# Four later rounds of a token routing: the threshold by sorting instead of by counting search, and a smaller first piece for the first expert

## The chip, the cores and the metric

The kernel runs on one core of one Trainium2 chip. The metric is the device time of the whole kernel in microseconds, as the median of several executions. A profile is one execution of its own; its times are counted from the first instruction (the span's start). The core has a matrix engine (TensorE, "PE" in the rows, with its weight loads as "PEld"), a vector engine (VectorE, "DVE"), a scalar engine (ScalarE, "ACT"), a general engine (GpSimd, "POOL") and an engine that here only issues transfers (SyncE, "SP"). Each runs its own list of instructions in order, and they meet at semaphores.

## The reference

```python
x = attention(q, k, v, f_logit)            # gated linear recurrence, then (3072 tokens, 384)
# routing and first network
cap = N // E                               # 3072 // 8 = 384
logits = x @ w_gate                        # (3072, 8)
for idx in np.argsort(-logits.flatten()):  # greedy, best logit first
    tok, e = idx // E, idx % E
    if assigned[tok] >= 0 or counts[e] >= cap: continue
    assigned[tok] = e; counts[e] += 1
for e in range(E):
    out[assigned == e] = np.maximum(x[assigned == e] @ w1[e], 0.0) @ w2[e]
# second network on every token: h = x @ w_in; g = h * clip(h + 3, 0, 6) / 6; y = g @ w_out
```

With 384 places in each of 8 experts and 3072 tokens, the greedy loop ends with every expert exactly full. The kernel computes the same assignment in rounds: every token picks the best expert that is left to it, every expert finds the logit of its 384th best token (its threshold), the tokens below it lose that expert and pick again. When no expert is over 384, the choice is the reference's.

## The kernel before

**Stages.** First the attention, in 24 units of 128 tokens, on all engines, with the weights of the second network split into a high and a low part beside it (chunks of 512 columns, loaded by SP, rounded by ScalarE, the rest subtracted by GpSimd). It leaves the 24 x 8 logits of each of the 128 lanes in `logit` (128 x 192). Then the routing. Then 8 experts one after the other, each with 384 gathered tokens: transpose, first network, second network, scatter of the result. Every product there is three matmuls (high x high, high x low, low x high; lines 1580 to 1582).

**A routing round** (`for r in range(COARSE)`, line 1238, four rounds with `DIGITS = (3, 3, 4, 4)`). `make_values` (L1099) writes to `vm` the logit of each token's choice and about -1e38 elsewhere. VectorE (L1104, tiles 0 to 8) and ScalarE (L811, tiles 9 to 23) copy `vm` to `vsel`, each value 16 times; TensorE turns the 24 tiles (`turn_values`, L1506), so that PSUM lane 16 e + j holds all 3072 values of expert e, for 16 trial keys j. Then comes the search, 3 or 4 digits of base 16 long. For each digit VectorE counts the values at or above the lane's key in the first 1408 columns (L1179), ScalarE in the other 1664 (L814), L1187 compares the sum with 384, a matmul (L1535) adds up the lanes' verdicts, and L1205 makes the next key. The last key is the threshold (`base`); `threshold` (L1521) brings it to all lanes. `limit_choice` (L1077, L1080) drops the logits under it, `choose` (L1086, L1089) finds each token's new best expert. From the second round on a search starts at the key found in the round before it, with a window of a 16th of the scale (`set_window`, L1129 to L1136).

TensorE also runs matmuls whose results nobody reads: `warm` (L1494, 128 columns each) and 16 others of 128 columns ahead of a round's last digit (L1533).

**After the rounds** `count_choice` (L1514, L1516) and `judge` (L1147 to L1174) count each expert's tokens and work out where each token stands in its expert's list. If an expert is still over 384, `exact_rounds` runs further rounds, with eight digits each, behind a flag that all engines read (`load_flag`). 24 matmuls (L1573) sum the row numbers, L1297 writes `ids`, and GpSimd gathers the rows of expert 0 in three indirect transfers of 128 rows (L682).

**Expert 0's start.** TensorE turns tile 0 as it lands (`first_turn`, L1597), ScalarE and VectorE split it in high and low (L864, L1306), then `first_hidden(0)` multiplies it with the first two 128-column blocks of w1 (18 matmuls of 128 columns). Only then are tiles 1 and 2 turned and split, and `first_hidden(1)` and `first_hidden(2)` follow, with 18 matmuls of 128 columns each. Afterwards `expert` goes on with `hidden(2)`, which waits for the first block's low part (`hl`, L1312, behind `hh`, L872).

**Weights of expert 0.** SP loads w1[0] (L544) when the attention's stores have landed and w2[0] (L547) when w1[0] has been split, both through one buffer `raw`. GpSimd splits both in six pieces of 512 columns (L671 and L673), with waits on `v_turned` that hold pieces back to the second and third round. `expert_split` must be through before `first_hidden`. The end of the kernel is GpSimd's wait for all 24 scatters (L721).

Of the kernel before, what the change touches and what calls it, by code (L numbers as in the profile page):

```python
# [4 lines left out]
F32 = mybir.dt.float32  # L5
# [3 lines left out]
I32 = mybir.dt.int32  # L9
U32 = mybir.dt.uint32  # L10
ALU = mybir.AluOpType
# [33 lines left out]
DIGITS = (3, 3, 4, 4)  # L45
WINDOW = 1.0 / 16.0
COARSE = len(DIGITS)
BEFORE = tuple(sum(DIGITS[:r]) for r in range(COARSE + 1))
COARSE_STEPS = BEFORE[COARSE]
# [4 lines left out]
def build(nc, q, k, v, f, wg, w1, w2, wi, wo, out):  # L54
    ctx = ExitStack()
    with ctx:
# [61 lines left out]
        bottom = place("acts", "bottom", [P, 1])  # L118
        wide_lane = place("acts", "wide_lane", [P, 1])
        window = place("acts", "window", [P, 1])  # L120
# [20 lines left out]
        count_from = place("acts", "count_from", [P, 1])  # L141
        count_a = place("acts", "count_a", [P, 1])
# [51 lines left out]
        vm = place("routing", "vm", [P, NT, NE])  # L194
# [43 lines left out]
        w2h = place("expert", "w2h", [P, F1 // P, DM], F32R)  # L238
        w2l = place("expert", "w2l", [P, F1 // P, DM], F32R)
# [11 lines left out]
        count_d, unread = psum[:, ND + 16:ND + 17], p7[:, 0:P]  # L251
# [4 lines left out]
        id_ps = p5[:, 0:NT]  # L256
        fT_ps, kT_ps, qT_ps = p0, p1, p2
# [75 lines left out]
        order_counted = sem("order_counted")  # L333
        placing = sem("placing")
# [7 lines left out]
        window_set = sem("window_set")  # L342
        moves_set = sem("moves_set")
# [4 lines left out]
        raw_loaded = sem("raw_loaded")  # L348
        high_done = sem("high_done")
# [130 lines left out]
        def exact_key(r):  # L480
            return (STEPS - 1) * (r - COARSE) + COARSE_STEPS - COARSE

# [3 lines left out]
        def _(sp):  # L486
# [52 lines left out]
            def weights(e):  # L539
                if first(e):  # L540
                    sp.wait_ge(chunk_split, NT)
                else:
                    sp.wait_ge(split_done, 2 * e)
# [6 lines left out]
            def exact():  # L550
# [13 lines left out]
                sp.wait_ge(scan_stored, 1 + 16 * NT)  # L564
            for i in range(B):
                sp.wait_ge(x_stored[i], 16 * TT)
# [3 lines left out]
            weights(0)  # L570
# [4 lines left out]
            experts(sp, expert)  # L575

        @block.gpsimd
        def _(pool):
# [11 lines left out]
            for i in range(MOST):  # L590
# [6 lines left out]
                               pattern=[[16, NE], [0, 16]], channel_multiplier=-1).then_inc(rc, 1)  # L597
            pool.memset(head[:, :], 0.0).then_inc(rc, 1)
# [57 lines left out]
            def split(q, high, low):  # L656

                pool.wait_ge(raw_loaded, 16 * q + 16)
                high = high.rearrange("p c n -> p (c n)")
                low = low.rearrange("p c n -> p (c n)")  # L660
                pieces = PIECES if q < 2 else 1
                size = 3072 // pieces
                for i in range(pieces):
# [3 lines left out]
                    if q == 0 and i == 4:  # L667
                        pool.wait_ge(v_turned, 2)
# [1049 lines left out]
```

## Time and profile before

| | |
|---|---|
| median of 3 runs | 885.61 us (885.39 to 890.78) |
| the profiled execution | 886.32 us |
| its span, first to last instruction | 883.8 us |
| TensorE busy | 825.5 us (93% of the span) |
| VectorE, ScalarE, GpSimd busy | 384.3, 346.7, 324.8 us |
| chain that ended last, by engine | PE 89%, DVE 6%, issue 2%, the rest 3% |

A row of the chain gives start, length and what ran (`x2` means two instructions merged). A row of a timeline gives start, busy time, engine, line, operation, output and inputs with their shapes, and in brackets how long the engine had been idle and what ended that. A fp32 matmul appears as two. "PEclk" is the clock that TensorE was granted, 1.00 being its upper level (2.4 GHz) and 0.50 its lower one (1.2 GHz); a number between them is a mean over both.

### The profile page before, as it was taken

What the parts mean: (1) busy time and instruction counts of PE and PEld (TensorE: products, weight loads), DVE (VectorE), ACT (ScalarE), POOL (GpSimd) and SP (SyncE); (2) the same over time, 40 slices, a digit from 0 to 9 for tenths busy, and PEclk for the clock granted to TensorE, in tenths of its full rate; (3) what the DMA queues carried; (4) which work ended last, traced back from release to release, by engine and by line L of the source; (5) the groups of instructions that cost most, each with busy time, mean ns of one, the idle gap of its engine ahead of it and who ended that gap; (6) DMA issues with size and microseconds to landing.
All of it is one profiled execution on the core that took longest, in us unless ns stands there. A gap on an engine that the chain in (4) does not pass through costs nothing.

```text
span 883.8 us, 15679 instructions
## 1 busy us (share of the span) xinstructions
PE 825.5 (93%) x6030; PEld 795.6 (90%) x6030; DVE 384.3 (43%) x717; ACT 346.7 (39%) x631; POOL 324.8 (37%) x249
## 2 busy tenths in 40 slices
PE   5999999965569999999999999999999999999995
PEld 4899989854459999999999999999999999999995
DVE  6778776556741442343143234324313322431331
ACT  4766766444521432333143233314323332432332
POOL 4676767634220522440161244116024422601001
PEclk8999999977679999999999999999999999999998
DMA  9999999322210221040121103012211200200000
GB/s 164 200 175 186 184 193 173 79 83 71 72 36 20 72 72 54 1 143 10 45 71 71 53 6 136 19 34 71 71 53 36 106 30 23 71 0 27 1 1 27
DMA packets 126806, 65.03 MB, mean 74 GB/s; under 512 B 102448, under 2 KB 119856, under 8 KB 126768
## 3 DMA queue, kind: packets, MB, share of 16 engines
q1 hardware_dynamic: 123696, 55.09, 28.8%
q0 software_dynamic: 3072, 9.44, 3.3%
q8 instruction: 24, 0.39, 0.2%
q14 instruction: 14, 0.11, 0.0%
HBM read 55.07 MB, written 9.44 MB: 73 GB/s over the span
## 4 chain that ended last, share of the span: by engine, by line
PE 89%; DVE 6%; issue 2%; SPq 1%; ACT 1%; DMA 1%; POOL 0%; DVEq 0%; POOLq 0%
PE psum L1580 23%; PE psum L1582 22%; PE psum L1581 22%; PE psum L1340 4%; PE psum L1392 3%; DVE junk L1179 3%; PE psum L1427 3%; PE psum L1442 2%; PE psum L1377 2%; PE psum L1506 2%; PE psum L1405 1%; PE psum L1435 1%; PE psum L1369 1%; SPq L499 1%; PE psum L1591 1%
## 5 line engine op out<-in xcount | busy, mean ns | idle before, releaser
L1322 DVE SCALAR_TENSOR_TENSOR psum<-rg,psum 128x384 f32<-128x384 f32 x128 | 72.0, 563 | 155.3 <-ACT rg L882 155.3
L882 ACT ACTIVATE rg<-psum,three 128x384 f32<-128x384 f32 x128 | 74.5, 582 | 153.1 <-PE psum L1582 153.1
L1580 PE MATMUL psum<-yh,w_high 128*128 128x384 f32 x384 | 130.7, 340 | 0.9
L1580 PE MATMUL psum<-w_high,gh 128*128 128x384 f32 x384 | 128.4, 334 | 0.3 <-DVE gl L1325 0.3
L1582 PE MATMUL psum<-yh,w_low 128*128 128x384 f32 x384 | 128.6, 335 | 0.0
L1581 PE MATMUL psum<-yl,w_high 128*128 128x384 f32 x384 | 128.5, 335 | 0.0
L1582 PE MATMUL psum<-w_high,gl 128*128 128x384 f32 x384 | 128.3, 334 | 0.0
L1581 PE MATMUL psum<-w_low,gh 128*128 128x384 f32 x384 | 128.3, 334 | 0.0
L716 POOL DMA_INDIRECT out_dram<-ys,ids x24 | 24.1, 1002 | 255.2 <-ACT ys L897 250.6
L1312 DVE SCALAR_TENSOR_TENSOR hl<-psum,hh 128x384 fp32r<-128x384 f32 x64 | 35.7, 558 | 166.2 <-ACT hh L872 166.2
L1325 DVE SCALAR_TENSOR_TENSOR gl<-psum,gh 128x384 fp32r<-128x384 f32 x128 | 71.4, 558 | 72.4 <-ACT gh L886 72.4
L886 ACT ACTIVATE gh<-psum 128x384 fp32r<-128x384 f32 x128 | 63.0, 493 | 81.5 <-DVE psum L1322 81.5
L872 ACT ACTIVATE hh<-psum 128x384 fp32r<-128x384 f32 x64 | 31.5, 492 | 146.3 <-PE psum L1582 142.8
L671 POOL CAST w1h<-raw 128x3072 fp32r<-128x3072 f32 (+1 forms) x13 | 22.9, 1764 | 145.0 <-PE psum L1582 125.8
L1580 PEld LDWEIGHTS psum<-yh,w_high 128*128 128x128 f32 x384 | 72.1, 188 | 4.3 <-DVE yl L1316 3.5
L1580 PEld LDWEIGHTS psum<-w_high,gh 128*128 128x128 f32 x384 | 72.1, 188 | 0.6 <-DVE gl L1325 0.6
L1581 PEld LDWEIGHTS psum<-yl,w_high 128*128 128x128 f32 x384 | 72.2, 188 | 0.0
L1582 PEld LDWEIGHTS psum<-w_high,gl 128*128 128x128 f32 x384 | 72.1, 188 | 0.0
L1581 PEld LDWEIGHTS psum<-w_low,gh 128*128 128x128 f32 x384 | 72.1, 188 | 0.0
L1582 PEld LDWEIGHTS psum<-yh,w_low 128*128 128x128 f32 x384 | 72.1, 188 | 0.0
L1580 PE MATMUL psum<-xh,w1h 128*128 128x384 f32 (+1 forms) x204 | 67.3, 330 | 1.8 <-DVE xl L1306 1.6
L1582 PE MATMUL psum<-xh,w1l 128*128 128x384 f32 (+1 forms) x204 | 67.2, 329 | 0.0
(191 smaller groups left out, 1616.1 us busy)
## 6 DMA issues: line engine op xcount, KB each, us to landing
raw<-in_moe_w_dram SPq DMA_DIRECT2D x16, 1536.0 KB, 6.5
f_in<-in_f_logit_dram SPq DMA_DIRECT2D x24, 192.0 KB, 4.6
k_in<-in_k_dram SPq DMA_DIRECT2D x24, 192.0 KB, 5.2
q_in<-in_q_dram SPq DMA_DIRECT2D x24, 192.0 KB, 5.5
v_in<-in_v_dram SPq DMA_DIRECT2D x24, 192.0 KB, 4.6
x_rows<-x_nat SPq DMA_DIRECT2D x24, 192.0 KB, 4.1
raw<-in_moe_w_in_dram SPq DMA_DIRECT2D x12, 256.0 KB, 4.3
raw<-in_moe_w_out_dram SPq DMA_DIRECT2D x12, 256.0 KB, 3.4
```

The costliest lines, as they stand in the source:

```text
L872: act.activation(hh[:, j % 2, :], banks[j % 2][:, 0:CAP], ACT.Relu).then_inc(hh_done, 1)
L882: act.activation(rg[:, j % 2, :], banks[j % 3][:, 0:CAP], ACT.Relu, bias=three[:, 0:1]).then_inc(r_done, 1)
L886: act.mul(gh[:, j % 3, :], banks[j % 3][:, 0:CAP], 1.0 / 6.0).then_inc(gh_done, 1)
L1179: dve.tensor_scalar(junk[:, :], v_dve, key, count_from[:, 0:1], ALU.is_ge, ALU.add, accum_out=count_d).then_inc(count_done, 1)
L1312: dve.scalar_tensor_tensor(out=hl[:, j % 2, :], in0=banks[j % 2][:, 0:CAP], scalar=0.0, in1=hh[:, j % 2, :].bitcast(F32), op0=ALU.max, op1 ...
L1322: dve.scalar_tensor_tensor(out=bank, in0=rg[:, j % 2, :], scalar=6.0, in1=bank, op0=ALU.min, op1=ALU.mult).then_inc(gg_done, 1)
L1325: dve.scalar_tensor_tensor(out=gl[:, j % 3, :], in0=bank, scalar=1.0 / 6.0, in1=gh[:, j % 3, :].bitcast(F32), op0=ALU.mult, op1=ALU.subtra ...
L1340: last = pe.transpose(dst[:, P * g:P * g + P], src[:, b, 2 * g:2 * g + 2, :].rearrange("p a b -> p (a b)"), ident[:, :])
L1392: last = pe.matmul(a_ps[j][:, P * g:P * g + P], k_sc[r, i, P * g:P * g + P], q_sc[r, i, P * g:P * g + P], start=True, stop=True)
L1580: pe.matmul(bank, high, rhs_high, start=start, stop=False)
L1581: pe.matmul(bank, high, rhs_low, start=False, stop=False)
L1582: return pe.matmul(bank, low, rhs_high, start=False, stop=stop)
```

## The change

Round 1 stays a search, with two digits instead of three. It is followed by four rounds of another kind (`RANKED = 4`; five rounds in all). In such a round `vm` holds the negated logit of the choice, and about -1e38 elsewhere, in 32 tiles (24 and 8 that are always empty). Four transposes without any widening turn it, two to bank 0 and two to bank 1 (`ranked_ps`, `ranked_too`), so that a lane holds 256 values of one expert. VectorE takes the eight largest of each lane (`dve.max`; the negated values make them the eight smallest logits), copies them to a 16 x 8 grid in which only the lane's own tile is not zero (`spread`), and a matmul with `lane_expert` collects the 128 candidates of each expert in one lane (`merged_ps`). A second `dve.max` sorts out the eight smallest of the expert. ScalarE counts each lane's chosen tokens with one pass over `ranked_too` (as printed), a matmul sums the lanes of an expert, and VectorE picks from the eight the entry that belongs to the number of tokens over 384. A round can so drop at most seven tokens of an expert. TensorE runs 9 matmuls of 512 columns per such round whose results nobody reads (`fill`).

Further parts: w1[0] is loaded as soon as the attention's chunks are split; w2[0] goes to a place of its own (`w2_raw`, over `w2l`) once round 1 has turned its values; its high part is made by ScalarE in the ranked rounds, two pieces in each of the first three, its low part by GpSimd. GpSimd reads the gathers' bound from a register that is set once. `first_hidden` multiplies tile 0 alone with block 0, then with block 1, then tiles 1 and 2 together. The wait for the last scatters goes from GpSimd to SP. Small tables are made at the kernel's start, and one of VectorE's table steps waits for them.

```diff
-DIGITS = (3, 3, 4, 4)
+DIGITS = (2,)
+SEARCHED = len(DIGITS)
+RANKED = 4
+W2_ROUND = ((0, 2), (2, 4), (4, 6), (6, 6))
...
 sp
-                if first(e):
-                    sp.wait_ge(chunk_split, NT)
...
+            sp.wait_ge(chunk_split, NT)
+            sp.dma_start(raw[:, :]..., w1[0:1, :, :]...).then_inc(raw_loaded, 16)
             for i in range(B):
                 sp.wait_ge(x_stored[i], 16 * TT)
...
-            weights(0)
+            sp.wait_ge(v_turned, 1)
+            sp.dma_start(w2_raw[:, :]..., w2[0:1, :, :]...).then_inc(w2_loaded, 16)
...
+            sp.wait_ge(stored, 48 * NE)
 pool
-                    if q == 0 and i == 4:
-                        pool.wait_ge(v_turned, 2)
-                    if q == 1 and i == 0:
-                        pool.wait_ge(v_turned, 3)
...
+            pool.reg_mov(last_row, NTOK - 1)
...
-                                            bounds_check=NTOK - 1, oob_is_err=False).then_inc(xs_loaded[t], 16)
+                                            bounds_check=last_row, oob_is_err=False).then_inc(xs_loaded[t], 16)
...
-            expert_split(0)
+            split(0, w1h[:, :, :], w1l[:, :, :])
+            for i in range(PIECES):
+                finish_w2(i)          # waits for w2_high, subtracts
+            pool.wait_ge(w2_low, PIECES)
+            pool.sem_inc(split_done, 1)
...
-            pool.wait_ge(stored, 48 * NE)
 act
+            act.wait_ge(rank_tables, 3)
+            for r in range(1, RANKED + 1):
+                act.wait_ge(ranked_turned_too, r)
+                act.activation(junk_a[:, 0:2 * P], ranked_too, ACT.Sign, scale=1.0, bias=half_big[:, 0:1],
+                               accum_out=lane_count[:, :]).then_inc(lane_counted, 1)
+                for i in range(*W2_ROUND[r - 1]):
+                    if i == 0:
+                        act.wait_ge(w2_loaded, 16)
+                    act.copy(w2h[...][:, at], w2_raw[:, at]).then_inc(w2_high, 1)
 dve
+            def make_ranked(r):
+                dve.scalar_tensor_tensor(out=flat(vm[:, :, :]), in0=low_ps, scalar=-BIG, in1=flat(logit[:, :, :]),
+                                         op0=ALU.mult, op1=ALU.subtract).then_inc(ranked_made, 1)
+            def rank(r):
+                dve.wait_ge(ranked_turned, r)
+                dve.max(out=top_ps, in_=ranked_ps).then_inc(top_done, 1)
+                dve.wait_ge(top_done, r)
+                dve.tensor_tensor(spread[...], top_ps..., lane_tile..., ALU.mult).then_inc(spread_done, 1)
+                dve.wait_ge(merged, r)
+                dve.max(out=least_ps[:, 1:RANKS + 1], in_=merged_ps).then_inc(sorted_done, 1)
+                dve.wait_ge(lanes_summed, r)
+                dve.tensor_scalar(code_ps, lane_sum_ps, rank_code_at(RANKS - 1), rank_code_at(-1), ALU.min, ALU.max).then_inc(code_done, 1)
+                dve.wait_ge(code_done, r)
+                dve.wait_ge(sorted_done, r)
+                dve.scalar_tensor_tensor(out=picked[:, :], in0=rank_code[0:NE, :], scalar=code_ps, in1=least_ps, op0=ALU.is_equal,
+                                         op1=ALU.mult, accum_out=least[:, :]).then_inc(least_done, 1)
...
-            for r in range(COARSE):
+            for r in range(SEARCHED):
                 make_values(r)
-                if r == 0:
-                    set_scale()
-                else:
-                    set_window(r)
+                set_scale()
+                ranked_constants()    # minus (8 x 8), and a memset of vm's empty tiles
                 coarse(r)
+                limit_choice(r)
+                choose(r + 1)
+            dve.memset(least_ps[:, 0:1], BIG)
+            for r in range(1, RANKED + 1):
+                make_ranked(r)
+                rank(r)
                 limit_choice(r)
                 choose(r + 1)
 pe
+            def rank(r):
+                fill(p4, 4 * P, 5)
+                pe.wait_ge(ranked_made, r)
+                ...
+                for dst_ps, done in ((ranked_ps, ranked_turned), (ranked_too, ranked_turned_too)):
+                    for i in range(2):
+                        last = pe.transpose(...)
+                    last.then_inc(done, 1)
+                fill(p4, 4 * P, 2)
+                pe.wait_ge(spread_done, r)
+                pe.matmul(merged_ps, lane_expert[:, :], spread[:, :], start=True, stop=True).then_inc(merged, 1)
+                pe.wait_ge(lane_counted, r)
+                pe.matmul(lane_sum_ps, lane_expert[:, :], lane_count[:, :], start=True, stop=True).then_inc(lanes_summed, 1)
+                fill(p4, 4 * P, 2)
+                pe.wait_ge(least_done, r)
+                pe.matmul(thr_ps, least[:, 0:1].broadcast_to([NE, P]), minus[:, :], start=True, stop=True).then_inc(t_ready, 1)
...
-            warm(16)
             pe.wait_ge(x_copied, NT)
+            fill(p0, 4 * P, 2)
             pe.wait_ge(measured, 2)
             pe.matmul(peak_ps, peak[:, 0:1], ident[:, :], start=True, stop=True).then_inc(peak_turned, 1)
+            fill(p0, 4 * P, 4)
...
-                    if i and i == DIGITS[r] - 1:
+                    if i:
                         pe.wait_ge(bits_ready, BEFORE[r] - r + i)
-                        for _ in range(16):
-                            pe.matmul(unread, ones_b[:, :], ones_b[:, :], start=True, stop=True)
+                    else:
+                        pe.wait_ge(scaled, 1)
+                    fill(p7, 3 * P, 8)
...
             first_turn(0)
-            warm_late(2)
-            pe.wait_ge(ids_known, 1)
-            pe.wait_ge(split_done, 2)
-            first_hidden(0)
             first_turn(1)
+            pe.wait_ge(split_done, 1)
+            first_hidden(0, 1, 0)
             first_turn(2)
-            first_hidden(1)
-            first_hidden(2)
+            first_hidden(0, 1, 1)
+            first_hidden(1, 3, 0)
+            first_hidden(1, 3, 1)
```

## Rows read from the trace of the kernel before

**Rows 1.** Windows: stretch, length, busy us (count) by engine, PEclk, DMA share, GB/s.
```profile
253.80:267.10 13.30, 10.02 (x83) 9.28 (x81) 2.14 (x4) 1.94 (x5) 6.25 (x6) 0.99 0.26 77
267.10:875.50 608.40, 606.64 (x3501) 602.11 (x3501) 201.15 (x364) 199.15 (x388) 174.66 (x68) 1.00 0.14 47
```

**Rows 2.** Chain that ended last, round 1, the start of round 2, and round 4's end.
```profile
187.96 1.82 DVE junk L1179 x2
...
190.57 1.82 DVE junk L1179 x2
...
193.20 0.61 PE psum L1521 x2
193.84 0.38 DVE psum L1077
...
196.23 4.44 PE psum L1506 x24
...
243.74 0.38 DVE psum L1077
```

**Rows 3.** Groups of VectorE in the routing, 178 to 253 us: busy, mean ns.
```profile
L1179 DVE TENSOR_SCALAR_CACHE_REDUCE junk<-psum,coarse_key,count_from 128x1408 bf16<-128x1408 f32 x10 | 17.4, 1744 | 0.4
...
L1077 DVE TENSOR_TENSOR psum<-logit_peak,psum 128x192 f32<-128x192 f32 x4 | 1.5, 364 | 2.8 <-PE psum L1521 2.8
...
L1086 DVE TENSOR_REDUCE psum<-logit_peak 128x24 f32<-128x192 f32 x4 | 1.4, 361 | 0.1
...
L1153 DVE TENSOR_REDUCE slotf<-incl 128x24 f32<-128x192 f32 x1 | 0.6, 615 | 0.0
```

**Rows 4.** Chain: four transposes, and the matmul that turns the peak.
```profile
174.97 0.66 PE psum L1369 x4
...
180.06 0.51 PE psum L1526 x2
```

**Rows 5.** Timeline of TensorE, the unread matmuls ahead of a last digit.
```profile
190.59 1.89 PE L1533 MATMUL psum<-ones_b 128*128 128x128 bf16 x16 [0.39 <-DVE coarse_key L1205]
```

**Rows 6.** Windows, columns as in rows 1: end of round 1, round 2's transposes, its first count.
```profile
189.70:196.20 6.50, 5.39 (x42) 4.28 (x42) 4.94 (x16) 2.13 (x3) 3.95 (x5) 0.50 0.00 0
196.20:199.80 3.60, 3.57 (x18) 3.57 (x19) 1.15 (x6) 1.59 (x3) 0.00 (x0) 0.54 0.02 5
200.00:203.20 3.20, 0.84 (x8) 0.53 (x5) 2.11 (x5) 1.74 (x2) 2.40 (x3) 0.96 0.00 0
```

**Rows 7.** Groups of ScalarE in 180 to 330 us: busy, mean ns.
```profile
L811 ACT COPY vsel<-vm 128x640 f32<-128x640 f32 x10 | 6.7, 722 | 10.5 <-DVE vm L1099 10.5
...
L886 ACT ACTIVATE gh<-psum 128x384 fp32r<-128x384 f32 x13 | 6.4, 493 | 8.2 <-DVE psum L1322 8.2
...
L814 ACT ACTIVATION_READ_ACCUMULATOR junk_a<-psum,coarse_key 128x1 f32 x10 | 1.9, 193 | 0.0
```

**Rows 8.** Timeline of GpSimd: first piece of w1[0], last piece of w2[0].
```profile
186.16 0.61 POOL L671 CAST w1h<-raw 128x512 fp32r<-128x512 f32 x1 [12.32 <-DMA raw<-in_moe_w_dram]
...
225.59 1.27 POOL L673 TENSOR_TENSOR w2l<-raw,w2h 128x512 fp32r<-128x512 f32 x1
```

**Rows 9.** Chain from the token lists to the first expert's steady work.
```profile
252.61 0.19 DVE ids L1297
...
253.77 3.40 DMA xs<-x_rows,ids
257.21 0.56 PE psum L1597 x3
...
259.01 0.30 PE psum L1580
...
265.98 0.50 ACT hh L872
...
267.12 0.44 PE psum L1580
267.56 0.17 PE psum L1581
```

More of the change, by code:

```diff
@@ L44 @@
 UNCHOSEN = 4096.0
-DIGITS = (3, 3, 4, 4)
[L46 to L49, printed above, removed]
+DIGITS = (2,)
+SEARCHED = len(DIGITS)
+RANKED = 4
+COARSE = SEARCHED + RANKED
+BEFORE = tuple(sum(DIGITS[:r]) for r in range(SEARCHED + 1))
+COARSE_STEPS = BEFORE[SEARCHED]
+LANE_TILES = 16
+RANKS = 8
+W2_ROUND = ((0, 2), (2, 4), (4, 6), (6, 6))
 MOST = max(DIGITS)
@@ L193, in build @@
         junk_a = place("routing", "junk_a", [P, NTOK - ND], BF16)
-        vm = place("routing", "vm", [P, NT, NE])
+        vm_all = place("routing", "vm_all", [P, 2 * LANE_TILES, NE])
+        vm = vm_all[:, 0:NT, :]
         vsel = place("routing", "vsel", [P, NT, NE, 16])
@@ L238, in build @@
         w2h = place("expert", "w2h", [P, F1 // P, DM], F32R)
+        top["w2 raw"], limit["w2 raw"] = top["expert"], limit["expert"]
+        w2_raw = place("w2 raw", "w2_raw", [P, F1 // P * DM])
         w2l = place("expert", "w2l", [P, F1 // P, DM], F32R)
@@ L250, in build @@
         digit_ps, thr_ps = p7[:, 384:385], p7[:, 392:392 + NE]
[L251 removed]
+        count_d = psum[:, ND + 16:ND + 17]
         def value_at(n):
@@ L842, in search @@
                 widen_rest(r)
-                act.wait_ge(v_turned, r + 1)
+                act.wait_ge(v_turned, turning(r) + 1)
                 for i in range(STEPS):
@@ L1176, in judge, with test @@
                                       ALU.is_equal).then_inc(columns_done, 1)
-            def test(key, m, starts=None):
+            def test(key, m):
                 dve.tensor_scalar(junk[:, :], v_dve, key, count_from[:, 0:1], ALU.is_ge, ALU.add,
                                   accum_out=count_d).then_inc(count_done, 1)
-                if starts is not None:
-                    size = scale if starts == 0 else window
-                    dve.tensor_scalar(move_ps, unit_move[:, :], size[:, 0:1], None, ALU.mult).then_inc(moves_set, 1)
-                    dve.wait_ge(moves_set, starts + 1)
+                if isinstance(m, int) and m == 0:
+                    dve.tensor_scalar(move_ps, unit_move[:, :], scale[:, 0:1], None, ALU.mult).then_inc(scaled, 1)
+                    dve.wait_ge(scaled, 4)
                 dve.wait_ge(count_done, m + 1)
@@ L1190, in coarse @@
             def coarse(r):
-                dve.wait_ge(v_turned, r + 1)
+                dve.wait_ge(v_turned, turning(r) + 1)
                 for i in range(DIGITS[r]):
@@ L1208, in search @@
             def search(r):
-                dve.wait_ge(v_turned, r + 1)
+                dve.wait_ge(v_turned, turning(r) + 1)
                 for i in range(STEPS):
@@ L1519, in threshold, with fill @@
             def threshold(r):
-                pe.wait_ge(base_done, r + 1)
+                pe.wait_ge(base_done, turning(r) + 1)
                 pe.matmul(thr_ps, base[:, 0:1].bitcast(F32).broadcast_to([P, P]), head[:, :], start=True, stop=True).then_inc(t_ready, 1)
-            warm(16)
+            def fill(bank, width, count):
+                rows_of_ones = ones_b[:, :].unsqueeze(1).broadcast_to([P, width // P, P])
+                for _ in range(count):
+                    pe.matmul(bank[:, 0:width], ones_b[:, :], rows_of_ones, start=True, stop=True)
```

154 lines of the change are left out of this document (102 added, 52 removed).

## Prediction

> **What bounds the kernel now.** The windows by stage come first: from 267.10 to the end of the last expert TensorE is busy 606.64 of 608.40 us at full clock [rows 1]. The change touches nothing in there that TensorE waits for, so that stretch stays. What is left to gain lies ahead of it, in the routing (178.6 to 252.8) and the first expert's start. There the chain that ended last is read, because busy shares say little in a stretch where three engines wait for one another: a round is a string of VectorE's counts, TensorE's small matmuls and the widened transposes [rows 2]. Then the groups of VectorE and ScalarE give prices by size [rows 3, 7], the windows tell the clock [rows 6], and the chain behind the token lists shows how the first tile comes in [rows 9].
>
> **Does it still end in time?** The number of tokens over capacity follows from the inputs, and the reference's logits give it in plain arithmetic. Before: the experts are over by at most 59 tokens, then 14, 7, 3 after rounds 1 to 3, and 0 after round 4; the chain has no exact round. After: at most 13 with the two-digit threshold, then 6, 2, 2, and 0 after the fourth ranked round. Although a ranked round drops at most seven tokens of an expert, five rounds suffice, with none to spare.
>
> **Rounds 2 to 5.** Before, from the moment `vm` of round 2 is made (195.80, which is 193.84 plus five vector instructions of 0.39 apart) to the first instruction after the last threshold (243.74) it takes 47.94 us [rows 2]. A ranked round from `vm` to the same place:
> - two transposes: four take 0.66 at full clock [rows 4]; I take 0.45, and 0.08 for two semaphores. Bounds 0.35 and 0.66.
> - `dve.max` over 128x256. No row shows it. A plain reduction of 192 takes 0.361, one of a strided 192 takes 0.615, and the slope from 192 to 1408 elements is (1.744 - 0.361) / 1216 = 1.14 ns [rows 3]. One pass over 256 would be 0.43; at the dearest row's price per element (3.2 ns) 0.82. It reads one contiguous stream, so I take the near row, 0.43 + 0.03.
> - `spread`, 128x128 with a broadcast: 0.364 less 64 x 1.14 ns is 0.29, + 0.03 [rows 3].
> - `merged`: an fp32 matmul over 128 columns is 0.51 [rows 4], with semaphores 0.61.
> - second `dve.max`, 8x128: 0.29 + 0.03 (dearest 0.41).
> - `code` 0.19, as a small vector instruction from PSUM [rows 9], and `picked` the same with 0.08 for its accumulator (an estimate; ScalarE's accumulator takes 0.193 [rows 7]), 0.27.
> - the threshold matmul, from key to L1077, 193.20 to 193.84 and 0.02 before: 0.66 [rows 2].
>
> Sum: 0.53 + 0.46 + 0.32 + 0.61 + 0.32 + 0.19 + 0.27 + 0.66 = 3.36. Between rounds stand five vector instructions 0.395 apart, 1.98. Four rounds: 4 x 3.36 + 3 x 1.98 = 19.4, and 0.1 for one memset. **Gain 28.4.** Bounds: 28.4 - 4 x (0.39 + 0.12 + 0.21) = 25.5 with the dear prices; at full clock the matmuls are shorter than the rows' (193.20 fell in a stretch at 0.50 [rows 6]), up to 0.3 a round, so 29.6.
>
> Beside the path: ScalarE's count over 128x256 is about 0.38 (0.493 for 384 less 128 x 0.9 ns) plus 0.193 for the accumulator [rows 7]; it starts some 0.3 after VectorE's `max` does and has 0.8 until `merged` starts, so it is hidden, narrowly. If it were not, it would cost what it is late, some tenths. Its two w2 copies follow, each about 0.61 (0.722 less 128 x 0.9 ns) [rows 7]; 1.2 us, behind which only the next round's count is queued, more than 3 us away.
>
> The Trainium skill (Vector Engine (DVE) Microarchitecture Reference, section 3.9) describes the eight-largest instruction as one stream through eight compare-and-swap cells, drained in eight cycles. By that the two `max` would cost 0.44 and 0.30, the near row's price; no row here shows it.
>
> **Round 1.** One digit less: 190.57 - 187.96 = **2.6** [rows 2]. New on VectorE are two small constants ahead of the count, on TensorE six unread matmuls of 512 columns around the peak's for 16 of 128, and eight of 384 under each count. At full clock 384 columns go by every 0.17 [rows 9], eight in 1.4, below the count's 1.74 + 0.14 of VectorE [rows 3]. At the lower clock 128 columns take 1.89 / 16 = 0.118 [rows 5], eight of 384 some 2.8, which would show by 0.9 each. I take 0 for all of it, bounds -0.3 and +2.
>
> **The first tile.** Before: tile 0 turned at 257.2, its two blocks from 259.01 to 261.0, tiles 1 and 2 only then, block 0's low part starting with `hh` at 265.98, `hidden(2)` at 267.12 [rows 9]. After: gathers land 1.3 to 1.6 apart, so tile 1 is turned at about 258.5 and tile 2 at 260.0, while tile 0 x block 0 (9 matmuls, 1.0) runs at 259.1. Tile 2's split is done at about 261.7; tiles 1 and 2 with block 0 are 9 matmuls of 256 columns, about 1.1, so `hh` starts at 263.1 instead of 265.98: **2.8**. Bounds 1.0 (a late third landing) and 3.3. `hidden(2)` still has the 1.14 us of `hh` and `hl` ahead of it, covered by the second block.
>
> **Moved work.** w1[0]'s first piece now waits for `v_turned` (184.8), not for its load (186.16) [rows 8]. Six pieces of 1.9 end near 196.3. w2[0] is loaded from 184.9, landing near 192; ScalarE first needs it near 194.5. Six subtractions of 1.27, paced by three ranked rounds, end near 208, against a first use near 233. Before they ended at 226.9 [rows 8] against 259. All hidden with 25 us of room; were it late, `hidden(2)`'s wait would take it up. SP is past both waits long before the next load can start. The tables at the start cost VectorE some 0.4 us in an idle stretch of 1.3 before the first scan. The register bound and the moved last wait: a few 0.1 us each, **0.4** together; bounds 0 and 2.
>
> **Sum.** 28.4 + 2.6 + 2.8 + 0.4 = 34.2. The profiled execution took 886.32, 0.7 above the median; against its own time it comes to 852.1, against the median 885.61 to **851.5**.
>
> **Rivals.**
> *A, the fills stand in the way.* If the clock stays low in the ranked rounds, five fills take 5 x 0.47 = 2.4 (four times 0.118 each) against 1.98 of VectorE, two behind the transposes with the second pair 1.3 against 0.8: with slower transposes 1.0 a round, and 0.9 on each of round 1's counts. 4 + 1.8: **857.3**. For it: 0.50 was granted over the end of round 1 although TensorE was busy 5.39 of 6.50 [rows 6]. Against it: that followed a stretch with little work, and after busy transposes (3.57 of 3.60, at 0.54) the next stretch had 0.96 [rows 6]. In the new rounds TensorE has some 3.3 us of work in 5.3 and no long gap. Chance 0.13.
> The Trainium skill (TensorE: Matmul & The Clock Gate, Part 4) says that transposes do not count as activity for the full clock. By it only the fills would hold the clock up and A would gain weight. The trace disagrees: 196.20 to 199.80 held transposes alone, and the clock rose behind it [rows 6].
> *B, `max` is dear.* At the dearest row's price 0.51 a round, 2.0 in all, and another 2 if spread and picked are dearer too: **855**. Chance 0.1.
> *C, the rounds do not suffice* (the other side). If logits computed on the chip leave one token over, one exact round runs: 0.4 + 4.4 for turning, 8 x 2.61 of digits, 0.66 + 1.6 and 8.9 for counting and placing again (243.74 to 252.61) [rows 2, 9], together 36.9: **888.4**, within 1% of before; a second makes 925. It decides as soon as one expert is over 384 after round 5. Against it: the arithmetic above ends at 0 for these inputs. Chance 0.03.
> *D, the change does not reach the end:* the gain would be lost if something other than `ids` set the gather. After the lists only w1 and the rows in memory are needed, both early. Chance 0.01, near 885.
>
> **How the numbers follow.** The forecast (849 to 854) has 0.73. The range 847.5 to 858 takes in A and B and the dear and cheap bounds singly; C, D and sums of dear bounds are left out. Faster by over 1% (8.9 us, about what a measurement can tell here) are the forecast, A and B: 0.96; within 1%: C's first case and D, 0.025; slower 0.015.
>
> **What would show it.** Four rounds of about 5.3 us between `make_ranked` instructions, `max` near 0.43 and 0.29; PEclk near 1.00 through them (A: near 0.5 and TensorE busy throughout); 2.6 less in round 1; `hidden(2)` some 7.1 us behind the first tile's landing, where it was 9.9 (257.21 to 267.12); no line of the exact rounds. It is wrong if a `max` takes over a microsecond, if the rounds are over 6.5 us, or if an exact round shows.

## The result, and the profile after

| | before | changed |
|---|---|---|
| median, us | 886.5 (885.39 to 890.78, 4 runs) | **844.49** (843.58 to 845.32, 4 runs) |
| profiled execution, us | 886.32 | 843.58 |
| its span, us | 883.8 | 841.8 |
| ratio of the medians | | 0.9517 (0.9483 to 0.9552) |

The change takes 42.0 us off the median and off the span. 851.5 was predicted, with 847.5 as the low end of the range: the sign was right, the time lies 3.0 us under the range, and the gain came out 7.8 us above the 34.2 of the sum. (The prediction started from 885.61, the median of three executions; with a fourth it is 886.5.) The page of the changed kernel, share of the span and instructions by engine, and the granted clock in 40 slices:

```profile
PE 809.2 (96%) x5869; PEld 775.1 (92%) x5869; DVE 360.9 (43%) x667; ACT 324.8 (39%) x612; POOL 322.4 (38%) x247
...
PEclk8999999999799999999999999999999999999999
```

The windows of the changed kernel, columns as in [rows 1]: ahead of round 1's first count, round 1, the four ranked rounds, the token lists, the gather with expert 0's start, and the experts.

```profile
177.60:182.65 5.05, 5.04 (x36) 3.71 (x37) 1.98 (x11) 2.01 (x4) 0.00 (x0) 1.00 0.81 303
182.65:188.36 5.71, 3.72 (x22) 1.76 (x21) 4.54 (x13) 3.44 (x4) 4.24 (x5) 1.00 0.77 257
188.36:207.90 19.54, 14.19 (x76) 6.57 (x74) 12.43 (x45) 5.33 (x14) 14.11 (x13) 1.00 0.13 35
207.90:216.78 8.88, 3.44 (x43) 2.71 (x44) 7.45 (x17) 3.89 (x10) 1.16 (x1) 0.62 0.29 118
216.78:227.70 10.92, 9.83 (x65) 9.02 (x65) 2.40 (x5) 2.05 (x5) 6.12 (x6) 0.84 0.29 82
227.70:836.10 608.40, 606.50 (x3501) 601.87 (x3501) 201.10 (x364) 198.84 (x388) 175.46 (x70) 1.00 0.14 47
```

Read against [rows 1], the last window is the same work in the same time. Everything gained lies ahead of it, apart from 2.35 us at the end, from the last scatter on. TensorE's share rose to 96% because most of the stretches in which it waited are gone, and unread matmuls fill part of the others; its clock in the ranked rounds is 1.00.

Cut at the same instructions in both traces, the two spans differ stage by stage like this (lengths in us):

| stage, up to | before | changed | gain | predicted |
|---|---|---|---|---|
| the attention's end | 178.58 | 177.61 | 0.97 | 0 |
| round 1's first count | 6.29 | 5.04 | 1.25 | 0 |
| the limit (first instruction behind round 1's threshold) | 8.97 | 5.71 | 3.26 | 2.6 |
| the limit behind the last threshold | 49.90 | 19.54 | 30.36 | 28.4 |
| `ids` written | 8.87 | 8.88 | 0 | 0 |
| the first gather's start | 1.16 | 0.47 | 0.69 | 0.4, all three together |
| tile 0 turned | 3.44 | 3.38 | 0.06 | 0 |
| `hidden(2)` | 9.91 | 7.10 | 2.81 | 2.8 |
| last copy to `ys` | 607.89 | 607.63 | 0.26 | 0 |
| last scatter's start | 1.81 | 1.28 | 0.53 | see above |
| end of the span | 6.98 | 5.16 | 1.82 | see above |

So the 7.8 us are 1.96 in the ranked rounds, 1.9 in round 1, 1.0 in the attention, 2.6 in the ends of the gather and the scatters, and 0.3 in the experts. All but the last were put to an experiment.

### The profile page after: what moved, and what is told of

It is laid out like the page before. It is cut to its first block, busy times and chain, and to the rows that moved or that the text cites. A ratio compares the mean times of both kernels' runs of the same rounds, so it can differ in the third digit from the quotient of the medians.

```text
span 841.8 us, 15206 instructions
## 1 busy us (share of the span) xinstructions
PE 809.2 (96%) x5869; PEld 775.1 (92%) x5869; DVE 360.9 (43%) x667; ACT 324.8 (39%) x612; POOL 322.4 (38%) x247
## 4 chain that ended last, share of the span: by engine, by line
PE 91%; DVE 4%; issue 1%; SPq 1%; ACT 1%; DMA 1%; POOL 0%; POOLq 0%; DVEq 0%; ACTq 0%
PE psum L1694 24%; PE psum L1696 23%; PE psum L1695 23%; PE psum L1430 4%; PE psum L1482 3%; PE psum L1517 3%; PE psum L1532 2%; PE psum L1467 2%; PE psum L1495 1%; PE psum L1525 1%; PE psum L1459 1%; PE psum L1705 1%; SPq L537 1%; DVE yl L1406 1%; ACT yh L948 0%
## 5 line engine op out<-in xcount | busy, mean ns | idle before, releaser
L1694 PE MATMUL psum<-xh,w1h 128*128 128x384 f32 (+2 forms) x198 | 65.8, 332 | 0.4 <-DVE xl L1396 0.2
L1696 PE MATMUL psum<-xh,w1l 128*128 128x384 f32 (+2 forms) x198 | 65.6, 331 | 0.0
```

The lines of the kernel that those rows point to most:

```text
L1694: pe.matmul(bank, high, rhs_high, start=start, stop=False)
L1696: return pe.matmul(bank, low, rhs_high, start=False, stop=stop)
```

## The first ranked round, step by step

The chain of the changed kernel, from the limit behind round 1's threshold to the one behind the first ranked threshold:

```profile
188.36 0.37 DVE psum L1151
...
189.95 0.36 DVE vm_all L1178
...
190.45 0.42 PE psum L1626 x2
190.90 0.45 DVE psum L1184
191.37 0.30 DVE spread L1186
191.72 0.40 PE psum L1631 x2
192.14 0.30 DVE psum L1189
192.55 0.23 DVE picked L1194 x2
192.83 0.40 PE psum L1636 x2
193.25 0.37 DVE psum L1151
```

A round has a period of 193.25 - 188.36 = 4.89. The vector instructions between rounds take 190.31 - 188.36 = 1.95 (predicted 1.98). The ranked part takes 2.94, where the prediction had 3.36:

| step | predicted | measured |
|---|---|---|
| two transposes and their semaphores | 0.53 | 0.59 |
| first `max` | 0.46 | 0.47 |
| `spread` | 0.32 | 0.35 |
| `merged` matmul | 0.61 | 0.42 |
| second `max` and `code` | 0.51 | 0.41 |
| `picked` | 0.27 | 0.28 |
| threshold matmul | 0.66 | 0.42 |

What had no row before was priced well: both `max` and `spread` are within 0.03. The two matmuls had rows and were priced too high by 0.19 and 0.24, because these rows come from stretches at the lower clock. (The transposes, whose row was at the upper clock, were priced 0.06 too low.) The window of the kernel before around the 0.51 of [rows 4] shows that clock:

```profile
179.90:180.60 0.70, 0.70 (x5) 0.18 (x4) 0.00 (x0) 0.60 (x1) 0.00 (x0) 0.50 0.00 0
```

The timeline of the changed kernel (VectorE, ScalarE, TensorE) shows the instructions themselves:

```profile
190.90 0.44 DVE L1184 MAX8 psum<-psum 128x8 f32<-128x256 f32 x1 [0.59 <-PE psum L1626]
...
192.14 0.30 DVE L1189 MAX8 psum<-psum 8x8 f32<-8x128 f32 x1 [0.48 <-PE psum L1631]
...
191.18 0.47 ACT L889 ACTIVATE junk_a<-psum,half_big 128x256 bf16<-128x256 f32 x1 [4.13 <-PE psum L1626]
...
188.18 1.24 PE L1616 MATMUL psum<-ones_b 128*128 128x512 bf16 x5
```

A `max` over 256 elements takes 0.44 and one over 128 takes 0.30. The Trainium skill (Vector Engine (DVE) Microarchitecture Reference) has it as one stream through eight compare-and-swap cells (section 3.9) whose eight results are drained in eight cycles (section 4.3). It gives no time; the prediction's estimate by it, the price of a plain pass and these cycles, was 0.44 and 0.30, and the trace agrees. ScalarE's count starts 0.28 behind the `max` and its lane sum is there before VectorE needs it, so it stays hidden. The five fills ahead of a round take 1.24 (predicted 2.4 at the lower clock) under 1.95 of VectorE's work.

## Experiments

Times are medians; the kernel before had medians of 886.7 to 891.1 beside them. Medians of the same kernel beside different runs differ by more than the smaller effects, so where less than 3 us is in question the stages of the table above are compared. Each stage is from one profiled execution of a kernel.

**The last wait goes back to GpSimd.**

```diff
 sp
-            sp.wait_ge(stored, 48 * NE)
 pool
+            pool.wait_ge(stored, 48 * NE)
```

> The changed kernel with one part undone: the wait for the last scatters stands on GpSimd again and not on SP. Theory 'the tail': in the profile the stretch from the last scatter's start to the end of the span fell from 6.98 to 5.16 us because of this move; then it is about 7.0 again here and the time 1.8 us higher (about 846.3). Rival 'the tail is chance' (a transfer that happened to land earlier): it stays at 5.2 and the time at 844.5.

Measured: 846.71 (845.98 to 847.16). From the last scatter's start to the end it is 6.95 again, where the changed kernel has 5.16 and the kernel before 6.98. The last scatters are unchanged, as the timeline of GpSimd shows, first for this kernel and then for the changed one:

```profile
838.25 0.98 POOL L777 DMA_INDIRECT out_dram<-ys,ids  x1 [0.30 <-issue]
```

```profile
836.64 0.97 POOL L778 DMA_INDIRECT out_dram<-ys,ids  x1 [0.30 <-issue]
```

The spans end at 845.2 and 841.8, 3.4 apart: 1.8 of it is the place of this one wait, and 1.7 is the stretch up to round 1's first count (6.71 instead of 5.04), of which more below.

**The bound as an immediate again.**

```diff
-                                            bounds_check=last_row, ...)
+                                            bounds_check=NTOK - 1, ...)
```

> The changed kernel with one part undone: the bound of the indirect transfers is a constant again and not a register set once. Theory 'the wake': GpSimd started the first gather 0.97 us after ids was ready before the change and 0.28 after it, and the last tiles' first scatter 0.79 and 0.28 us after ys; the move that precedes each transfer is the cause; then both gaps return and the time is 0.7 + 0.5 = 1.2 us higher. Rival (the earlier part of GpSimd's code decides): the gaps stay at 0.28, no difference.

Measured: 847.50 (846.85 to 848.53). The chain of this kernel behind the lists:

```profile
218.45 0.19 DVE ids L1385
...
218.69 0.67 issue
...
219.40 0.20 issue
219.61 0.36 POOL xs L732
```

From `ids` to the gather 1.16, where the changed kernel has 0.47; the stretch from the last copy to the last scatter's start is 1.80 instead of 1.28. 0.69 + 0.52 = 1.2 us hang on the bound. That GpSimd spends this time, between its wait and the transfer, on setting the bound is the likely reading; a trace shows only "issue" there. It is paid by the first transfer behind a wait: the next one follows after an idle time of 0.30 in both kernels.

**Both ends alone, in the kernel before** (register bound, last wait on SP, nothing else of the change).

> The kernel before with two parts of the change alone: the bound in a register, and the last wait on SP. Theory: 1.2 + 1.8 = 3.0 us less than before (886.5 to 883.5), if the two ends are additive and do not hang on the rest. Rival: under 1 us.

Measured: 885.01 (883.38 to 887.77, 10 runs), ratio 0.9967 (0.9949 to 0.9986). Stages against before: gather 1.16 to 0.48, last scatters 1.81 to 1.27, end 6.98 to 5.19, together 3.0. The two parts stand by themselves and are worth the same in either kernel. The median moved by only 2.3; the stages are cut around the edited places and hold nothing else that was edited.

**No unread matmuls in the ranked rounds.**

```diff
             def rank(r):
-                fill(p4, 4 * P, 5)
...
-                fill(p4, 4 * P, 2)
...
-                fill(p4, 4 * P, 2)
```

> The changed kernel without the 9 unread matmuls in each ranked round. Theory 'the clock': they hold TensorE's clock at its upper level, so without them the granted clock falls to 0.5 within the first ranked rounds, and each round's small matmuls (0.42 + 0.40 + 0.40 us on the chain) go to about 0.55 + 0.51 + 0.61, as such matmuls took at the lower clock before: 0.45 us a round, about 1.5 to 1.8 in four, and the first tile may lose more. Rival 'the fills do nothing': the clock stays, and the time too; rival A of the prediction (the fills are in the way) would make it faster by up to 4 us.

Measured: 847.41 (846.76 to 848.19); the four rounds take 21.95 instead of 19.54. In the chain of this kernel, the transposes, the merge and the threshold of the second ranked round, behind the first round's transposes:

```profile
192.56 0.42 PE psum L1625 x2
...
197.86 0.67 PE psum L1625 x2
...
199.37 0.61 PE psum L1629 x2
...
200.69 0.60 PE psum L1633 x2
```

and its windows, one at the start of the rounds and one in the midst of them:

```profile
188.00:193.00 5.00, 2.16 (x14) 1.16 (x12) 3.46 (x11) 1.16 (x2) 4.84 (x6) 1.00 0.58 213
198.00:204.00 6.00, 2.75 (x13) 1.99 (x14) 3.10 (x11) 1.59 (x4) 3.23 (x3) 0.50 0.00 0
```

Without fills the clock falls to the lower level in the first ranked round and stays there, and the three steps take 0.67 + 0.61 + 0.60 instead of 0.42 + 0.40 + 0.40: 0.66 more, of which 2.41 / 4 = 0.60 show. The expectation had 1.5 to 1.8 in all; the mechanism holds, its size was too low. This is the explanation of the first 1.96: the prediction had priced a round as this kernel runs it. 28.4 predicted against 49.90 - 21.95 = 27.95 here.

**Round 1 with the old unread matmuls.** The six of 512 and the eight of 384 columns per count give way to `warm(16)` and 16 of 128 columns ahead of the last digit.

> The changed kernel with TensorE's unread matmuls of round 1 as they were before (16 of 128 columns ahead of the peak, 16 of 128 ahead of the last digit, none elsewhere); the ranked rounds keep theirs. Theory 'the clock': the transposes of round 1 run at a mixed clock again (4.3 us for 24 instead of 3.1), the threshold matmul at 0.61 instead of 0.40: 1.3 + 0.2 + 0.4 = about 1.9 us more. Rival: round 1 was shorter by other things (its first digit had a gap of 0.45 us behind its small matmul that is gone) and the time hardly changes, under 0.5.

Measured: 845.97 (845.84 to 846.45). Round 1 takes 6.01 instead of 5.71, and the first ranked round 0.26 more. Up to the first count it takes 7.53, but the sibling kernels that keep the wide fills show 6.5 to 8.0 there, so this can't be laid to the edit. About 0.6 us are left for the edit; the +1.9 that was expected were too many.

That stage also holds the 1.25 us that the profiled execution gained ahead of the first count. The chain of the changed kernel there, and that of the kernel with the last wait on GpSimd, which has the same code up to this place:

```profile
178.53 0.97 PE psum L1616 x4
179.50 2.07 PE psum L1596 x19
```

```profile
178.24 1.48 PE psum L1617 x4
179.72 3.23 PE psum L1597 x19
```

The same matmuls take 3.04 or 4.71. In the one execution TensorE's clock stayed at 1.00 from its wait behind the attention up to the count; in the other it stood at 0.50 from 179 to 181. The 5.04 is an exception: all nine other profiled kernels that keep the wide fills here show a fallen clock and take 6.47 to 7.97 for this stage, while the five kernels built on the one before that keep the old unread matmuls take 6.09 to 6.38 (and the one with wide fills 6.76). So this stage's 1.25 is the luck of one execution, and what the wide fills do in it is more likely a loss than a gain. The medians may have a share of this luck: two kernels further down that differ from the changed one only in where tiles lie had 845.91 and 845.22 beside its 844.49.

**Three digits in round 1.**

```diff
-DIGITS = (2,)
+DIGITS = (3,)
```

> The changed kernel with three digits in round 1 instead of two. Theory: a digit is 2.6 us at either clock, because VectorE's count is its bulk: 847.1, and all of it in round 1. Rival: the fills under the count make a digit dearer, over 3.

Measured: 848.15 (847.48 to 849.31). Round 1 takes 8.32 instead of 5.71: a digit costs 2.61 here, exactly what [rows 2] gave. The 3.26 gained in this stage are a digit, 0.2 of threshold at the upper clock (0.40 for 0.61), and a gap of 0.45 behind the first digit's small matmul ("issue" in the chain of before) that is not in the chain after. The gap is in all six kernels built on the one before, also in that with the wide fills, and in none built on the changed one, also not in that with the old unread matmuls. So it isn't the fills that took it away; what did was not found out.

**Wide fills in the search rounds of the kernel before** (before with the new fills in all four rounds, nothing else).

> The kernel before with wide unread matmuls in its four search rounds (8 of 384 columns under every count, 1 of 512 four times between rounds, 2 and 4 of 512 around the peak), nothing else changed. Theory 'the clock': transposes of a round go from 3.4 to 4.4 us to about 2.9, the threshold matmul from 0.61 to 0.40; about 1.3 + 1.5 + 0.6 + 0.6 + 4 x 0.2 = 4.8 us less. Rival: the clock follows the transposes alone and the time stays.

Measured: 887.95 (884.38 to 889.77, 10 runs), ratio 0.9999 (0.998 to 1.0018). Rounds 2 to 4 take 49.32 instead of 49.90. The windows of this kernel on the three stretches of widened transposes:

```profile
197.50:202.10 4.60, 4.56 (x26) 4.49 (x27) 1.16 (x6) 1.62 (x4) 0.00 (x0) 0.63 0.01 4
212.90:215.80 2.90, 2.90 (x26) 2.82 (x27) 1.13 (x6) 1.59 (x4) 0.00 (x0) 1.00 0.00 0
229.20:233.40 4.20, 4.18 (x26) 4.11 (x27) 1.14 (x6) 1.58 (x3) 0.00 (x0) 0.67 0.85 349
```

In the chain these transposes take 4.52, 2.85 and 4.18, where before they took 4.44, 3.52 and 3.45: one stretch of three ran at full clock, and the sum is no better. Expert 0's start and its experts took 2.8 more in this execution. The wide fills by themselves take nothing measurable off the search rounds: the gain is the sorting, and the fills keep it whole.

**The old order of expert 0's start.** `first_hidden` by tiles as before, all of the rest as changed.

> The changed kernel with the first expert's old order (tile 0 with both blocks before tiles 1 and 2 are turned, all in pieces of 128 columns, and the wait for the whole split). Theory: the order alone is worth the 2.8 us that were predicted and seen between the first tile's landing and hidden(2) (9.9 to 7.1): about 847.3. Rival: the landing of the tiles was what changed, and the order is worth under 1.

Measured: 849.78 (single executions 850.94, 848.62, 847.42 and 851.0). Up to `hidden(2)` it takes 11.14, where the kernel before took 9.91 and the change 7.10, and the experts take another 1.8. The windows of this kernel:

```profile
225.00:229.00 4.00, 3.17 (x29) 2.93 (x28) 1.02 (x2) 0.86 (x2) 1.67 (x2) 1.00 0.10 20
229.00:232.00 3.00, 3.00 (x21) 3.00 (x20) 0.00 (x0) 0.45 (x1) 1.33 (x2) 0.65 0.51 153
232.00:236.00 4.00, 4.00 (x16) 4.00 (x16) 1.11 (x2) 0.54 (x2) 0.00 (x0) 0.50 0.06 19
```

TensorE is busy without a gap from 228 on, and yet its clock fell at 230 and stood at 0.50 up to 236.7, into `hidden(2)` and beyond. Ahead of that lie the two gaps of some 0.8 that the old order leaves while a tile is split. That these gaps brought the fall is argued from this one execution; the kernel before has them too, and in its profile the clock stays at 1.00 there.

**The new order alone, in the kernel before.**

> The kernel before with the new order of the first expert's tiles alone. Theory 'the order': 2.8 us less in the stretch from tile 0's turning to hidden(2). Theory 'the clock falls in the first expert' (with the old order under the new rounds it fell there to 0.5 for some 7 us, and the time of single executions lay at 847.4 or at 851): the executions of the kernel before near 890.5, one in four, are of that kind, and with the new order they are gone. Rival: the high executions stay, one in four, 4 us above the others.

Measured: 883.96 (883.38 to 885.45, 12 runs), ratio 0.9967 (0.9954 to 0.998). Up to `hidden(2)` it takes 7.02 instead of 9.91: 2.9, the order's own gain, as in the changed kernel. And something that no stage of one profile can show: the kernel before ran 23 times beside this one, and six of these took over 889.5 (up to 892.15); the highest of this kernel's twelve is 885.45. The kernel above, changed with the old order, splits in the same way, and its profiled execution shows the clock fallen in expert 0's start. That the six of the kernel before have the same cause is likely, but none of them was profiled. Nor is the new order proof against it: in the kernel with fills under the token lists, below, the clock stood at 0.50 from 224 to 234 with the new order.

**Where the loads land: by 32 bytes.** The attention ends 1.0 us earlier after the change, which edits nothing there. The views of the transfers show what differs, first before, then changed; packets, MB, share of 16 engines, and under it KB and median us from issue to landing:

```profile
f_in<-in_f_logit_dram SPq DMA_DIRECT2D x24, 192.0 KB, 4.6
```

```profile
q1 hardware_dynamic: 123696, 55.09, 24.5%
...
f_in<-in_f_logit_dram SPq DMA_DIRECT2D x24, 192.0 KB, 3.8
```

The same packets take less time: the 98304 packets of 192 bytes take 22.6 ns on average before and 15.4 changed. The change adds small tables to SBUF ahead of the attention's inputs, so these lie elsewhere. Two kernels put 32 bytes more in front:

```diff
+        place("acts", "shift_by_32", [P, 8])
```

> The kernel before with one change: the tiles of the attention (q_in, k_in, f_in, v_in and what follows) lie 32 bytes further on in SBUF; the change had moved them by 864 bytes, so that q_in began at 32768 instead of 31904. Theory 'the addresses': the 192-byte packets that fill them cost 22.6 ns before and 15.4 after the change, because they now begin at multiples of 64 bytes; then they cost about 15.4 here, and the first unread matmul behind the attention comes at about 177.5 instead of 178.6 to 179.6: about 1.6 us less. Rival 'something else in the start' (tables, the order of SP's list): 22.6 ns and no difference.

> The changed kernel with the same tiles shifted by 32 bytes, off the multiples of 64. Theory 'the addresses': 22.6 ns a packet and about 1.6 us more, all of it in the attention. Rival: 15.4 ns and no difference.

Measured: 886.78 (885.53 to 890.86) and 845.91 (844.96 to 846.46), packets 21.6 and 15.4 ns. Nothing moved, and the theory that the start must be a multiple of 64 bytes fell. A kernel with every area of the changed one on 64 bytes was no better either:

> The changed kernel with every area moved by 32 bytes, so that the raw weights, xs and ys, too, begin at multiples of 64 bytes, and a pad ahead of x_nat that keeps the attention's tiles where they are. Theory 'the addresses' for larger packets: the gathers (1536-byte rows) land a little sooner, 0.1 to 0.3 us in the first tile's path; nothing in the experts' stretch, which waits for no transfer. 844.2, the same as the change within what can be measured.

Measured: 845.22 (844.21 to 846.77), packets 15.5 ns.

**By 96 bytes.** What was left: per head 192 bytes are written, the heads of `q_in`, `k_in` and `f_in` lie 256 bytes apart, and `q_in` begins 160 bytes into a block of 256 bytes before the change and 0 after it. (`v_in` packs its heads without a gap, so some of its packets cross an edge at any place.) The 32 bytes moved that to 192 and 32: still across a block's edge in the one, still inside the block in the other. 96 bytes more swap the two.

> The kernel before with the attention's tiles 96 bytes further on, so that q_in, k_in and f_in begin at multiples of 256 bytes and each head's 192 bytes lie within one block of 256. Theory 'blocks of 256': the 192-byte packets cost 15.4 ns instead of 22.6 (at 160 bytes into a block, and at 192 with the shift by 32, they cross into the next one), and the attention ends 1.0 to 1.6 us sooner: 885.3. Rival 'not the addresses': 22.6 ns, no difference.

> The changed kernel with the same tiles shifted by 96 bytes, so that each head's 192 bytes cross into the next block of 256 (the shift by 32 did not make them cross). Theory 'blocks of 256': about 22 ns a packet, the attention 1.0 to 1.6 us longer. Rival: 15.4 ns and no difference.

Measured: 885.45 (883.42 to 888.74) and 847.19 (846.22 to 848.27). The transfers of the kernel before with 96 bytes more, and of the changed kernel with 96 bytes more:

```profile
q1 hardware_dynamic: 123696, 55.09, 23.3%
...
f_in<-in_f_logit_dram SPq DMA_DIRECT2D x24, 192.0 KB, 3.7
```

```profile
q1 hardware_dynamic: 123696, 55.09, 30.4%
...
f_in<-in_f_logit_dram SPq DMA_DIRECT2D x24, 192.0 KB, 4.6
```

Packets 15.4 and 22.9 ns, and the attention ends at 176.94 (with the old places 178.6 to 179.6) and at 178.62 (with the new ones 177.1 to 178.1). Both went the way that the block's edge demands. At the attention's end it is worth 0.5 to 2.7 us between single executions; in the medians (885.45 beside 886.91, 847.19 beside 844.49 of another time) it points the same way and is hardly above what they vary by. That the edge and nothing else about the place decides rests on these two pairs and on the two shifts of 32.

**Fills under the token lists** (the areas on 64 bytes, and 15 more fills of 512 columns around the counting of the tokens).

> The same, and 5 unread matmuls of 512 columns ahead of the counting of the choice and 10 behind it, in a stretch where TensorE idles and the clock fell in every profile so far. Theory 'the clock': the count and order matmuls start their followers about 0.15 sooner, and the 16 unread ones and the 24 that sum the row numbers go at full clock; VectorE's last column piece ends at the same time as before, so the lists gain 0.2 to 0.3 and the first tile as much again where its transposes waited for unread ones. 843.8. Rival: a fill in the way, slower by up to 0.5.

Measured: 847.02 (844.95 to 851.28). The lists take 8.85 as before, and in this execution the clock fell in expert 0's start (10.31 instead of 7.10 up to `hidden(2)`). Its six executions lie between 844.95 and 851.28. No version had a lower median than the change.

## Why the prediction came out as it did

The mechanism was right; sizes of the sum were wrong. Its failing terms are the ranked rounds (28.4 for 30.36, because two matmuls were priced at the lower clock) and the two ends (0.4 for 3.04). A term of 0 stood for the attention, which gave 1.0, and round 1 with the stretch ahead of it gave 1.9 more than the 2.6, of which 1.25 was luck. Without that luck the time would be near 845.7, still under the range.

- **What bounds it: right.** The experts take 608.40 in both windows. All of the gain lies ahead of them and at the end.
- **The number of rounds: right.** No line of the exact rounds ran, four ranked rounds stand in the trace. Rival C did not come.
- **Rounds 2 to 5: the mechanism right, 28.4 predicted, 30.36 measured.** The failing terms are `merged` (0.61 for 0.42) and the threshold (0.66 for 0.42). Both prices come from [rows 2, 4], which stand in stretches granted 0.50 (the window above, and [rows 6]), although the prediction itself held that the clock would be high in the new rounds and named "up to 0.3 a round" for that, in the bounds and not in the sum. A sum has to be made at one clock throughout. Most of the rest is `code`, which runs largely under the second `max` (the two take 0.41, not 0.51), and the memset (0.1), which is off the path; the transposes were priced a little low. The kernel without fills confirms it from the other side: at the lower clock the rounds take 21.95 and the gain would have been 27.95.
- **Rival A: wrong way.** It had the fills as a danger to the path. They are what holds the clock, and save 2.41 us. The evidence weighed against it pointed the right way: the clock stayed at 1.00 through all four rounds. The Trainium skill (TensorE: Matmul & The Clock Gate, Part 4) has transposes as no activity for the full clock; the runs speak against that as [rows 6] did. In the first window of the kernel with wide fills TensorE ran nothing but transposes from 197.5 to 201.8; the clock stood at 0.50 from 198 to 201 and rose to 1.00 by 201.4, while they still ran.
- **Rival B: did not come.** `max` costs the near row's price.
- **Round 1: 2.6 predicted, 3.26 measured**, and 1.25 ahead of it. The digit is right to 0.01. Missed were again the clock (0.2) and a gap of 0.45 in the search that the changed kernel no longer has; the 1.25 is one execution's luck, against which nine sibling profiles stand.
- **The first tile: right**, 2.8 predicted, 2.81 measured, and 2.9 when made alone. Missed was that the clock can fall in this stretch, as it did in one profile with the old order and in one with the new.
- **The ends: the failing term, 0.4 for 3.04.** The prediction called both edits a few tenths. For the register a row could have told: from `ids` at 252.61 to the gather at 253.77 in [rows 9] 1.16 us pass, of which `ids` itself is 0.19. The other 0.97 was the most that the edit could bring there; it brought 0.69. For the last wait no row of before gave a price; the 6.98 from the last scatter's start to the end could have been all transfer. Bounds of 0 and 2 were too narrow for two edits of which one had no row.
- **The start: predicted 0, measured 1.0.** "VectorE's tables in an idle stretch" was right and beside the point: what the tables changed was the place of everything behind them, and this moved the attention's inputs off a block's edge.
- **The range.** The misses were small and nearly all pointed the same way. The cheap bounds named in the text add up to 29.6 + 2.9 + 3.3 + 2 = 37.8, which is 847.8 against the median: still above 844.49. So it was not only that they were taken singly; the bounds themselves were too near, first those of the ends (2 for 3.04) and of the start (none for 1.0).

## What to carry to other kernels

Price every step of a stretch at the clock that the stretch will have, not at that of the row it is taken from, and keep it: a chain of small matmuls between vector instructions ran 12% longer without nine unread matmuls a round under it. An edit for which the trace has no row gets a bound from the whole wait that it could remove, even if it looks like housekeeping: the last wait's engine and a bound in a register were worth 3.0 us, as much as the reordering of the first tile. And if a new table shifts what lies behind it, look at where the transfers now land.

## What the runs showed of the hardware

- The instruction that finds the eight largest costs about as much as a plain pass over its input: 0.44 us for 128x256, 0.30 for 8x128, where the estimates from rows of plain instructions were 0.43 and 0.29.
- In the ranked rounds a small fp32 matmul, or two transposes, take 0.60 to 0.67 in the chain at the lower clock and 0.40 to 0.42 at the upper one.
- The first indirect transfer behind a wait came 0.69 us (the gather) and 0.52 us (the scatters) later with a constant bound than with the bound in a register.
- Ending the kernel in GpSimd's wait for the scatters took 1.8 us longer than ending it in SyncE's. Why was not found out.
- Where the 192-byte writes to `q_in`, `k_in` and `f_in` crossed the edge of a 256-byte block of SBUF, all packets of that size took 21.6 to 22.9 ns on average; where they did not, 15.4 to 15.5. Shown in both directions, by 96 bytes; 32 bytes, which moved no write across an edge, changed little.
- The same code ahead of the first count took 5.04 us with the clock at 1.00 throughout and 6.47 to 7.97 in nine profiles where the clock fell behind the attention or in the fills.
- In one profile TensorE's clock fell in the midst of work: it went from 1.00 to 0.50 2.4 us after the last gap (0.83 us long), and stood at 0.50 for 6.8 us in which the engine was busy throughout.
